# Weights loaded two experts ahead, the low half of h awaited pair by pair, and unused products on TensorE before the first expert

## The reference, cut to what matters

```python
attn  = softmax(where(q_assign == k_assign, q @ k.T * scale, -1e9)) @ v      # 16 heads, clusters as mask
x     = attn as [1536 tokens, 512]
e_of  = argmax(normalised x @ normalised expert_emb.T / tau)                 # one of 8 experts per token
for e in range(8):                                                           # middle layer, 512 -> 1024 -> 512
    out[e_of == e] = gate * (maximum(x[e_of == e] @ w1[e], 0) @ w2[e])
result = ((out @ w_a) * (out @ w_b)) @ w_out                                  # last layer, 512 -> 1536 -> 512
```

## Time and profile before

| | us |
|---|---|
| median of three runs | 911.27 |
| the profiled execution | 909.49 |
| its span | 907.7 |
| attention, logits, ranks (to 362.7) | 362.7 |
| TensorE idle between ranks and x (362.7 to 388.8) | 26.1 |
| eight experts (first product 392.0 to last 600.8) | 208.8 |
| last layer (603.8 to the end) | 303.9 |

### The profile page before, as it was taken

One profiled execution on the slowest core, in us unless ns is written; L12 is line 12 of the kernel. 1 busy time (PEld: TensorE's weight loads), 2 busy tenths in 40 slices (PEclk: granted clock), 3 DMA queues, 4 the chain that ended last, 5 costly groups with the idle time before them and its releaser, 6 DMA issues.

```text
span 907.7 us, 13554 instructions
## 1 busy us (share of the span) xinstructions
PE 824.3 (91%) x5377; PEld 738.3 (81%) x5378; DVE 417.0 (46%) x676; ACT 289.6 (32%) x499; POOL 106.1 (12%) x116
## 2 busy tenths in 40 slices
PE   5799999999999998077899999989999999999996
PEld 4589999999999994067899899878888888888885
DVE  5746776677766624232555544544413211131111
ACT  3123333333333355023445454534312111121111
POOL 6001221122112110630000000000000100010001
PEclk9999999999999999579999999999999999999999
DMA  4212332333322124443666656552000100010001
GB/s 132 53 40 71 99 86 72 81 104 97 78 63 64 51 94 140 142 124 126 209 207 207 207 187 205 176 176 93 1 0 1 47 1 1 0 47 1 1 1 46
DMA packets 61661, 80.06 MB, mean 88 GB/s; under 512 B 17992, under 2 KB 38696, under 8 KB 61600
## 3 DMA queue, kind: packets, MB, share of 16 engines
q1 hardware_dynamic: 59296, 72.90, 26.6%
q0 software_dynamic: 2304, 6.31, 1.8%
HBM read 57.11 MB, written 14.17 MB: 79 GB/s over the span
## 4 chain that ended last, share of the span: by engine, by line
PE 85%; issue 7%; DVE 3%; DMA 2%; SPq 1%; ACT 1%; another core or an unknown queue 0%; POOL 0%; POOLq 0%; ACTq 0%; DVEq 0%
PE bank L1190 14%; PE bank L1382 7%; PE bank L1384 7%; PE bank L1383 7%; PE pair L1148 5%; PE pair L1335 3%; PE pair L1337 3%; PE pair L1336 3%; PE first_pair L1174 3%; PE bank L1125 3%; PE first_pair L1176 2%; PE bank L1121 2%; PE first_pair L1401 2%; PE first_pair L1400 2%; PE first_pair L1399 2%
## 5 line engine op out<-in xcount | busy, mean ns | idle before, releaser
L1190 PE MATMUL bank<-v_sb,prob 128*128 128x66 f32 x1152 | 143.7, 276 | 0.0
L1190 PEld LDWEIGHTS bank<-v_sb,prob 128*128 128x128 f32 x1152 | 143.1, 196 | 0.1
L824 DVE TENSOR_REDUCE neg_max<-pair 128x1 f32<-128x768 f32 x93 | 88.7, 954 | 67.3 <-PE pair L1148 67.1
L1382 PE MATMUL bank<-x_hi,wt 128*128 128x512 f32 x288 | 112.7, 391 | 2.9 <-DVE x_lo L1056 2.9
L1384 PE MATMUL bank<-x_hi,wt 128*128 128x512 f32 x288 | 112.5, 391 | 0.0
L1383 PE MATMUL bank<-x_lo,wt 128*128 128x512 f32 x288 | 112.5, 391 | 0.0
L1078 DVE TENSOR_TENSOR g_sb<-bank,a_sb 128x512 f32<-128x512 f32 x36 | 24.9, 692 | 176.0 <-PE bank L1384 176.0
L566 ACT ACTIVATE prob<-first_pair 128x384 f32<-128x384 f32 x128 | 59.5, 489 | 128.3 <-PE first_pair L1176 127.7
L944 DVE TENSOR_TENSOR wt<-w_raw,wt 128x2048 fp32r<-128x2048 f32 x41 | 93.6, 2284 | 6.3 <-ACT wt L633 6.3
L1335 PE MATMUL pair<-ht_hi,wt 128*128 128x240 f32 x256 | 71.9, 281 | 12.9 <-DVE ht_lo L1019 12.9
L633 ACT ACTIVATE wt<-w_raw 128x2048 fp32r<-128x2048 f32 x41 | 78.1, 1906 | 3.3 <-DMA w_raw<-in_moe_w_dram 3.3
(11 more groups left out here) (212 smaller groups left out, 1579.9 us busy)
## 6 DMA issues: line engine op xcount, KB each, us to landing
w_raw<-in_moe_w_dram SPq DMA_DIRECT2D x32, 1024.0 KB, 8.5
x_slots<-out_sb SPq DMA_DIRECT2D x15, 512.0 KB, 3.7
q_raw<-in_q_dram SPq DMA_DIRECT2D x16, 192.0 KB, 2.4
k_raw<-in_k_dram SPq DMA_DIRECT2D x16, 192.0 KB, 2.5
v_sb<-in_v_dram SPq DMA_DIRECT2D x16, 192.0 KB, 3.1
qb<-qa SPq DMA_DIRECT2D x16, 192.0 KB, 2.6
kc<-kd SPq DMA_DIRECT2D x16, 192.0 KB, 2.9
w_raw<-in_moe_w_a_dram SPq DMA_DIRECT2D x3, 1024.0 KB, 11.2
```

The costliest lines, as they stand in the source:

```text
L824: dve.tensor_reduce(neg_max[n % 2][:, t:t + 1], masked_in(n, t)[:, :, 0:HALF], AX.XY, ALU.max, negate=True).then_inc(mx_done, 1)
L1190: last = pe.matmul(o_tiles[:, t, :], prob[s][:, j, t * P:(t + 1) * P], v_in_sb[u][:, j, :], start=(j == 0 and t == 0), stop=(j == NT - 1), ...
L1382: pe.matmul(to[:, :], w[0], x2_hi[:, kk, :], start=(kk == 0), stop=False)
```

## The change

SyncE issues the weights of expert e+2 during tile e: chunks 0 and 1 when all banks of h of expert e are complete (`h_full` at its end value), chunks 2 and 3 when the tile's last output block is complete (`y_full`). Expert 1's chunks are loaded before the loop, two before SyncE's wait for `scattered` and two behind the first `load_slots`. ScalarE and VectorE split all four chunks of expert e+1 during tile e, and expert 0's before the loop. TensorE's wait for the low half of h becomes four waits, one at each even `ff` of `d == 0`. And TensorE issues 84 matmuls on constants with 512 bf16 columns after `slots_ready`, waits for `scattered`, and issues 18 more; nothing reads their output.

```diff
@@ SyncE
             for c in (1, 2, 3):
                 load_chunk(0, c, c)
+            for c in (0, 1):
+                load_chunk(1, c, 4 + c)
             sp.wait_ge(scattered, 16 * TT)
             load_slots(0)
+            for c in (2, 3):
+                load_chunk(1, c, 4 + c)
             def expert(e, par):
                 first, end = base_of(sp, e, WINDOWS - 1), base_of(sp, e + 1)
                 load_slots(first + 1)
-                sp.wait_ge(h_full, HB * first + 1)
-                for c in range(4):
-                    load_chunk(e + 1, c, 4 * (1 - par) + c)
                 rest_of_expert(sp, first, end, lambda g: load_slots(g + 1))
+                n = e + 2
+                if not isinstance(e, int):
+                    sp.to_reg(n)
+                sp.wait_ge(h_full, HB * end)
+                for c in (0, 1):
+                    load_chunk(n, c, 4 * par + c)
+                sp.wait_ge(y_full, 2 * end)
+                for c in (2, 3):
+                    load_chunk(n, c, 4 * par + c)
...
             sp.dma_start(meta_back[:], ...).then_inc(meta_in, 16)
-            sp.wait_ge(y_full, 2 * base_of(sp, E))
-            for c in range(4):
-                load_chunk(E + 1, c, 4 + c)
             load_chunk(E + 2, 0, 8)
@@ ScalarE
-            for c in (1, 2):
+            for c in (1, 2, 3):
                 high_chunk(0, c, c)
             def tile(g, col, e=None, par=None):
                 relu(g, 0)
                 if e is not None:
-                    high_chunk(e, 3, 4 * par + 3)
+                    high_chunk(e + 1, 0, 4 * (1 - par))
                 relu(g, 1)
-                relu(g, 2)
-                if e is not None:
-                    high_chunk(e + 1, 0, 4 * (1 - par))
-                relu(g, 3)
                 if e is not None:
                     high_chunk(e + 1, 1, 4 * (1 - par) + 1)
+                relu(g, 2)
+                relu(g, 3)
                 x_high(g + 1)
+                if e is not None:
+                    high_chunk(e + 1, 2, 4 * (1 - par) + 2)
                 take_y(g, 0, col)
                 if e is not None:
-                    high_chunk(e + 1, 2, 4 * (1 - par) + 2)
+                    high_chunk(e + 1, 3, 4 * (1 - par) + 3)
                 take_y(g, 1, col)
@@ VectorE
             dve.tensor_copy(y_pos[:], pos_f[:]).then_inc(meta_ready, 1)
+            low_chunk(0, 2, 2)
+            low_chunk(0, 3, 3)
             def tile(g, e=None, par=None):
                 ht_low(g, 0)
-                if e is not None:
-                    low_chunk(e, 2, 4 * par + 2)
                 ht_low(g, 1)
                 if e is not None:
-                    low_chunk(e, 3, 4 * par + 3)
+                    low_chunk(e + 1, 0, 4 * (1 - par))
                 ht_low(g, 2)
                 ht_low(g, 3)
                 if e is not None:
-                    low_chunk(e + 1, 0, 4 * (1 - par))
+                    low_chunk(e + 1, 1, 4 * (1 - par) + 1)
                 x_low(g + 1)
                 if e is not None:
-                    low_chunk(e + 1, 1, 4 * (1 - par) + 1)
+                    low_chunk(e + 1, 2, 4 * (1 - par) + 2)
+                    low_chunk(e + 1, 3, 4 * (1 - par) + 3)
@@ TensorE
-            def down(slots, d):
+            def down(slots, d, g):
                 for ff in range(FT):
+                    if d == 0 and ff % 2 == 0:
+                        pe.wait_ge(ht_lo_done, HB * g + HB + ff // 2 + 1)
...
-                        if d == 0:
-                            pe.wait_ge(ht_lo_done, HB * g + HB + HB)
...
+            def keep_warm(times):
+                for _ in range(times):
+                    pe.matmul(bank[3][:, :], ones_bf[:], upper_bf[:, None, :].to_broadcast([P, 4, P]), start=True, stop=True)
+
             pe.wait_ge(slots_ready, 1)
+            keep_warm(84)
+            pe.wait_ge(scattered, 16 * TT)
+            keep_warm(18)
             turn_slots(0)
             experts(pe, expert)
```

More of the change, by code:

```diff
@@ L713, in _ @@
                     n = FFT * c + f
[L714 to L718, removed]
+                    if n in (2, 3, 4, 5):
                         high_chunk(E + 1, n - 2, n + 2)
@@ L1060, in _ @@
                 x2_low(0, kk)
-            low_chunk(E, 2, 2)
             dve.wait_ge(meta_in, 16)
@@ L1066, in _ @@
                     n = FFT * c + f
-                    if n == 1:
-                        low_chunk(E, 3, 3)
-                    elif n in (2, 3, 4, 5):
+                    if n in (2, 3, 4, 5):
                         low_chunk(E + 1, n - 2, n + 2)
@@ L1353, in tile @@
                             pe.wait_ge(w_lo[2 + d // 2], e + 1)
-                        if d == 0:
-                            pe.wait_ge(ht_lo_done, HB * g + HB + HB)
                         if d % 2 == 0:
                             pe.wait_ge(y_taken, 2 * g + d // 2 + 1)
-                        down(4 * par, d)
+                        down(4 * par, d, g)
                         if d == 0:
```

## The result

The changed kernel took 946.43 us in the median of four runs (945.65 to 955.48), the kernel before 912.37 beside it: ratio 1.039, 95% interval 1.033 to 1.046. The forecast was 898 us. The profiled execution has a span of 944.0 us. Some executions of a kernel take over 1.5% longer than its fastest; the ratios leave these out, the medians in the table of experiments do not (e7's mixes three of 891 to 899 with three of 912 to 923), and the one trace of e8 is of such an execution.

A forecast was written before the change was run, and what follows sets the result against it. The prediction took TensorE, on the chain of waits for 85% of the span, as the bound. Terms -10.0 - 2.9 - 1.1 + 1 = -13.0 against 909.49 gave 896.5, in the median 898 us; range 893 to 906.

The forecast's parts named there:

- Change of expert: Between experts, TensorE's program fetches would share the DMA engines with weights now issued there: +1 us, bounds 0 and +4.5.
- rival (a): The expert loop, touching 8 instruction blocks instead of 7, no longer stays on TensorE: 908.7 us, chance 0.09.
- Unused products: Before the first expert, products warm TensorE's clock: start +1.5 us, warm clock -3.0, taken as -1.1 of 0 to -3.
- Pair by pair wait: In `down`, waiting for h's low half in pairs closes a 1.43 us hole in seven tiles: -10.0 us.
- Chunks split one tile earlier: ScalarE's and VectorE's weight splits fit within each tile, and expert 0's into idle time before the loop: 0.
- The loads don't delay x: Before the first expert, expert 1's early weight loads leave x's arrival unchanged.
- First tile: In tile 0, expert 1's earlier loads remove the whole hole before `down`: -2.9 us.
- Last layer: At the last layer's start, the 2.92 us hole and its clock fall stay: 0, up to +1 us.
- (b): Before the first expert, TensorE stays at 1.2 GHz through all unused products, starting it 20.8 us later: 920 us, chance 0.04.
- (c): Within `down`, the pair wait moves the hole instead of closing it, giving back half of 10.0: 903 us, chance 0.07.

The follow-up runs named there:

- e7: The kernel before with only the four waits for pairs of h in place of one: 905.4 us, ratio 0.985 to the kernel before.
- e8: The changed kernel with the one wait for all of h and without the 102 unused products, so only weights and splits earlier: 912.5 us, ratio 0.999.
- e1: The changed kernel without the 102 unused products and their wait for the scatters of x: 896.2 us, ratio 0.984 to the kernel before.
- e2: The changed kernel with 26 tiny matmuls (52 instructions) more ahead of the 84 products: 908.6 us, ratio 0.997 to the kernel before.
- e3: The kernel before with 102 tiny matmuls (204 instructions) added ahead of the first turn of x, nothing of the change: 944.7 us, ratio 1.034.
- e6: The changed kernel with 50 tiny matmuls (100 instructions) in place of the 102 unused products and their wait: 923.8 us in one run, no ratio.
- e11: e2 with GpSimd's 12 scatters of gates and token numbers spread over the experts: 893.7 us, ratio 0.986 to the kernel before.
- e12: e1 with GpSimd's 12 scatters of gates and token numbers spread over the experts: 893.4 us, ratio 0.984 to the kernel before.
- e15: The changed kernel with only GpSimd's 12 scatters of gates and token numbers spread over the experts: 928.7 us, ratio 1.018 to the kernel before.
- e14: e2 without the 18 products behind the wait, 44 tiny matmuls in front keeping the loop's place: 896.0 us, ratio 0.984 to the kernel before.
- e5: e2 with SyncE issuing expert 1's chunks 2 and 3 only once x's first window is transposed: 907.5 us, ratio 1.000 to the kernel before.
- e9: e1 with TensorE's wait for the scatters of x kept: 899.0 us, ratio 0.991 to the kernel before.

## Why the prediction was wrong

**The step that failed** is "Change of expert", "+1, bounds 0 and +4.5". It took the holes for fetches, rightly, took for granted that the loop still stays on the engine, and asked only what weights beside the fetches would cost. Measured were +33.8 us of idle time at the changes of expert (40.28 against 6.44). What it did ask about was sized well: where the loop stays and lies alike, these holes sum to 8.0 us with the weights ahead (e1) and 7.3 without (e7). The count that shows why stood under rival (a): 204 instructions ahead of the loop move it from 7 blocks to 8. e2 and e3 show that the loop's place is the cause, in both directions. The error of judgement was the chance, 0.09, on "nothing shows that 8 are too many": nothing showed that 8 were few enough either, and the only case on record was 7.

**The price of rival (a) was wrong too,** 10.4 us. It took the holes of a first turn, 2 to 3.2 us, for a miss. Turning back costs 9.5 to 13.8 us, with three blocks in the hole of the changed kernel. The Trainium skill, "Runtime: NRT & Kernel Launch", Instruction fetch mechanics, says that a taken branch to a target outside the current window of two blocks has to fetch it first: the traces agree that there is a stall, with these numbers, but not on the window, since the loops of e1 and e2 stayed on 7 blocks. By the 2048 instructions that it gives TensorE a loop on 8 blocks should stay; e3, e6 and the changed kernel show that it doesn't, and the measurement decides.

**"Unused products"**: start +1.5 and clock -3.0 were forecast. The products themselves ran as worked out (102 in 24.5 us, clock up after 5 us, end at 390.3 where 391.7 was forecast). The start was +12.9: 10.0 from completions seen late, 2.9 from x. The prediction saw the same hold-up in tile 0 of the kernel before (400.79), and let it only take back the gain of the warm clock; that it could fall on the chain between x and the first product, where nothing covers it, was not thought of. Without it (e11 against e12) the start is +1.3 and the whole 1.1 us shorter, against 1.5 (1.1 taken) in the forecast; the times don't show it.

**"Pair by pair wait"** was right: no hole in any `down` of the changed kernel, -12.9 with tile 0, and 10.9 us for it alone in e7 against 10.0 plus up to 1.4.

**"Chunks split one tile earlier"** at 0 was right for the tiles, not for the start. That the splits of expert 0 "fall into 366 to 390, where both are idle" asked only whether VectorE is free, not what runs beside it: two of GpSimd's scatters took 2.4 us longer in all, and x's load was issued 2.3 us later. "The loads don't delay x" fails with it as a forecast of when x comes, though the loads themselves were not shown to do it. "First tile", -2.9, was right for its hole, which is gone in e1; 1.2 of it the pair wait takes by itself (2.91 to 1.67 in e7), the weights ahead the rest. The two nearly cancel in e8, 0.999.

**"Last layer"** at 0 was right within 1.3 us: 302.6 against 303.9. Of the rivals (b) and (c) nothing was seen.

With only the fetches away the time is 908.6 (e2), no gain over the kernel before and just above the range; with only the hold-up away it is 928.7 (e15), far above it. With both away it is 896.0 (e14) and 893.7 (e11), where 898 was forecast: the other terms held in sum, which is in part luck, since the late x was not among them and e11 also has its scatters spread.

## What to carry to other kernels

Count the program of a loop in blocks of 256 instructions, with its place, before adding or removing anything ahead of it: one that is fetched once or every turn differed here by 4% for 52 instructions of no work. In a profile the sign is instruction packets inside the loop's later turns and holes of no cause at its turn; the cheap test is to shift the loop and look again. Small scattered DMAs should not be bunched beside a hand-over between engines: spread over work that covers them they cost nothing here. And an engine that is idle can still slow another: two splits moved into VectorE's free time made x 2.3 us late. Moving them behind the scatters was not tried.

## What the runs showed of the hardware

- A loop of 1,675 to 1,687 instructions of TensorE stayed on the engine on 7 blocks (20.15 to 26.75, 21.15 to 27.75) and was fetched every turn on 8 (20.55 to 27.14, 20.95 to 27.5), in every case by the count.
- A turn back to a block no longer there cost 9.5 to 13.8 us of idle time, the other changes of expert in these kernels 0.2 to 3.8.
- The end of the first four transposes was seen 7.8 to 10.6 us late by ScalarE (e5, e2, changed), and by SyncE at the same time (401.49 and 401.52 in e5): 3.2 to 3.3 us after GpSimd had issued the last of 12 scatters of 128 8-byte rows. It stood only with the scatters bunched and products issued right behind a wait's release.
- GpSimd's issue of a scatter took 1.9 to 2.4 us where it began while a `low_chunk` of VectorE was running, and otherwise 0.96 (the first one 1.1), in all 17 traces.
- What the clock does behind a hole is not settled by its length: it was at 1.2 GHz 0.8 us behind one of 1.96 us in e9, and stayed at 2.4 GHz behind one of 3.40 us in e1. The two stretches, of e9 and of e1:

```profile
449.90:453.30 3.40, 3.40 (x18) 3.40 (x18) 0.00 (x0) 0.00 (x0) 0.00 (x0) 0.50 1.06 356
```

```profile
423.40:427.00 3.60, 3.57 (x31) 3.58 (x32) 0.00 (x0) 0.58 (x2) 0.00 (x0) 1.00 1.05 357
```
